# A gate part's phases summed and wrapped at its full length, a fold in two operations, a mask in one

## The chip, the cores and the metric

The kernel runs on one core of a Trainium2 chip. The metric is the device time in microseconds (us) of one execution. Its engines are TensorE (PE, matmul and transpose; its weight loads are PEld), VectorE (DVE), ScalarE (ACT), GpSimd (POOL) and SyncE (SP), which issues the DMAs. Each runs its own list of instructions in order, and they wait for one another through semaphores.

## The reference

Three stages follow one another: a gated linear attention with a complex gate, a token and channel mixer through a Fourier transform, and a second mixer with learned matrices. The change lies in the first and in the transform.

```
def _attn_ref(q, k, v, a_re, a_im):          # (4, 8, 768, 48) each
    mag = np.sqrt(a_re * a_re + a_im * a_im)
    scale = np.minimum(mag, 0.999) / (mag + 1e-06)
    a_re_n, a_im_n = (a_re * scale, a_im * scale)
    for t in range(S):
        new_re = ar * S_re - ai * S_im
        new_im = ar * S_im + ai * S_re
        S_re, S_im = (new_re + kv, new_im)
        y[:, :, t] = np.einsum('bhd,bhde->bhe', q[:, :, t], S_re)

def _moe_ref(x, w_ch1, w_ch2):               # x (4, 768, 384)
    X = np.fft.fft(np.fft.fft(x, axis=1), axis=2)
    u = x + np.real(X).astype(np.float32)
    un = (u - mean(u)) / np.sqrt(var(u) + 1e-06)
    return u + np.maximum(un @ w_ch1, 0.0) @ w_ch2

def _moe2_ref(x, w_tok1, w_tok2, w_ch1, w_ch2):
    u = x + (np.maximum(x.T @ w_tok1, 0.0) @ w_tok2).T
    return u + np.maximum(u @ w_ch1, 0.0) @ w_ch2
```

## The kernel before

The first stage works in chunks of 128 tokens. There are NM = 24 of them, six for each of four batches, numbered m, with j the place in the batch. In a chunk PE turns the keys (L1165, `turn_keys`), multiplies keys and queries into the scores of eight heads (L1173, four heads to a PSUM bank), adds to the state (L1202, `update`), and for the chunk before it multiplies the masked scores with the values (L1189) and the queries with the state (L1191). The outputs are turned (L1210, `turn_y`) and gathered into `yT`. Once a batch is whole its Fourier transform runs between the chunks: `middle` (L1219), `width_transform` (L1234) and `sequence_transform` (L1248 to L1252). `keep_busy` (L1258) issues matmuls with no use for their result: six at the very start, five in each chunk of the first batch and eight at the start of each later one. After chunk 23 come the two channel stages, whose matmuls are L233 to L235.

The gates are prepared ahead of this by ACT and DVE in nine parts, p0 to p8: p0 holds one chunk, p1 two, the others three each. A part holds 3 x 128 x chunks elements in each of 128 partitions, so 384, 768 or 1152. The magnitude of the gate gives the decays; its angle gives the phases. For the angle, ACT takes the arctangent and the sign of the real part (`arctangents`, L726 and L727) and writes with L730 into `t4` the half turn that is added where the real part is negative: 0.25 - 0.25 x sign, so 0 or 0.5. DVE (`phases`) scales the arctangent (L930) and then sums the angles over the tokens, a chunk at a time: three scans of 128 (L942), the nearest integer (L945), the difference, which is the wrapped phase (L947). The next chunk's scans start at the last value of the chunk before. L949 keeps the last value for the next part (`carry`). ACT takes the sines and cosines (`sines`, L737 to L740), and DVE multiplies keys and queries with them (`products`, L960 to L964); SP sends these out to memory and back in another layout (`turn_out`, `turn_back`), from where PE takes them.

The order on each engine is written out by hand. From p2 on, a part is spread over six chunks: squares in the first, magnitudes, inverses and factors, arctangents and phases in the fourth, sines and the first products in the fifth, the rest of the products in the sixth, with two chunks left before PE needs the part. In the fourth of these chunks `phases` stands on DVE ahead of `masked(m)`, which multiplies the scores of the chunk with the mask out of PSUM (L989, twice 512 elements), and `wait_for_outputs` makes PE wait for both halves before the next chunk's first L1189. On ACT, `arctangents` stands ahead of `keys_turned` (L746, which copies turned keys that PE needs for L1202), and `sines` ahead of it too; `magnitudes` stands ahead of `evacuate_y` (L753) and of `middle` (L765). `fold_sequence` on DVE adds and subtracts the two halves of a finished batch, for each of three groups (L1002, L1003), ahead of `width_transform`.

Of the kernel before, what the change touches and what calls it, by code (L numbers as in the profile page):

```python
# [8 lines left out]
B, H, S, D = 4, 8, 768, 48  # L9
# [3 lines left out]
P = 128  # L13
NT = S // P
KD = DM // P
# [10 lines left out]
fp32 = mybir.dt.float32  # L26
fp32r = mybir.dt.float32r
ALU = mybir.AluOpType
ACT = mybir.ActivationFunctionType
# [10 lines left out]
ROUND = 12582912.0  # L40
# [258 lines left out]
def forward(nc, ap, lay, c, u_out, x2, out, steep):  # L299
    with ExitStack() as ctx:  # L300
# [39 lines left out]
        GA = 16  # L340
        GV = [10 + 3 * p.chunks + 2 * len(PAIRS[p.n]) for p in parts]
        act0 = [GA * p.turn for p in parts]
# [67 lines left out]
        half_pi, ln_eps, ones = in_late(P, 1), in_late(P, 1), in_late(P, 1)  # L410
        least, at_floor, quarter, nearly_zero = in_late(P, 1), in_late(P, 1), in_late(P, 1), in_late(P, 1)
        bottom = in_late(P, 3 * TM)

# [23 lines left out]

        bank = [ctx.enter_context(nc.psum_tensor(f"bank{i}", [P, 512], fp32)) for i in range(8)]
        tr_bank, sc_bank, st_bank, y_bank, f_bank = bank[0:2], bank[2:4], bank[4], bank[5], bank[6:8]
# [43 lines left out]
        def products_done(p, i):  # L483
            return vec0[p.n] + 10 + 3 * p.chunks + 2 * (i // 2)

        def angles_room(p):
            return slice(2 * CT, 3 * CT) if p.n == 0 else slice(0, p.T)

# [195 lines left out]
        def _(act):  # L684
# [10 lines left out]
            def magnitudes(p):  # L695
                s, T, n = p.s, slice(0, p.T), act0[p.n]
                act.wait_ge(vec_step[s], vec0[p.n] + 1)
                A(t1_b[s][:, :, T], t1_b[s][:, :, T], ACT.Ln).then_inc(act_step[s], 1)
                act.wait_ge(act_step[s], n + 3)
                A(t2_b[s][:, :, T], t1_b[s][:, :, T], ACT.Exp, scale=-0.5, bias=ln_eps[:, 0:1]).then_inc(act_step[s], 1)  # L700
                if p.turn:
                    for m in range(parts[p.n - 2].first, parts[p.n - 2].end):
                        act.wait_ge(k_out[m % RING], 32 * (m // RING + 1))
                A(t3_b[s][:, :, T], t1_b[s][:, :, T], ACT.Exp, scale=0.5).then_inc(act_step[s], 1)
                for o in parts[max(p.n - 2, 0):p.n] if p.n > 1 else []:
                    act.wait_ge(vec_step[o.s], vec0[o.n] + 7 + 3 * o.chunks)
                A(t4[:, :, angles_room(p)], re_b[p.r][:, :, T], ACT.Abs).then_inc(act_step[s], 1)
# [15 lines left out]
            def arctangents(p):  # L723
                s, T = p.s, slice(0, p.T)
                act.wait_ge(vec_step[s], vec0[p.n] + 6)
                A(t3_b[s][:, :, T], t3_b[s][:, :, T], ACT.Arctan).then_inc(act_step[s], 1)  # L726
                A(im_b[p.r][:, :, T], re_b[p.r][:, :, T], ACT.Sign, scale=3.0,  # L727
                  bias=nearly_zero[:, 0:1]).then_inc(act_step[s], 1)
                act.wait_ge(act_step[s], act0[p.n] + 12)
                A(t4[:, :, angles_room(p)], im_b[p.r][:, :, T], ACT.Identity, scale=-0.25,  # L730
                  bias=quarter[:, 0:1]).then_inc(act_step[s], 1)

            def sines(p):
                s, T, n = p.s, slice(0, p.T), act0[p.n]
                re, im = re_b[p.r], im_b[p.r]
                act.wait_ge(vec_step[s], vec0[p.n] + 9 + 3 * p.chunks)
# [39 lines left out]

            act.wait_ge(consts_set, 4)
            logarithm_tables()
# [94 lines left out]
        def _(dve):  # L873
# [51 lines left out]
            def phases(p):  # L925
# [5 lines left out]
                                       op0=ALU.mult, op1=ALU.mult).then_inc(vec_step[s], 1)  # L931
                first = angles_room(p).start
                for i in range(p.chunks):
                    T = slice(i * CT, (i + 1) * CT)
                    offset = slice(first + i * CT, first + (i + 1) * CT)
                    dve.wait_ge(vec_step[s], n + 9 + 3 * i)
                    for g in range(3):
                        if i:
                            start = t3_b[s][:, g, i * CT - 1:i * CT]
                        else:  # L940
                            start = carry[:, 1 - s, g:g + 1] if p.j0 else 0.0
                        last = V.tensor_tensor_scan(t3_b[s][:, g, T], t3_b[s][:, g, T], t4[:, g, offset], start, ALU.add, ALU.add)  # L942
                    last.then_inc(vec_step[s], 1)
                    dve.wait_ge(vec_step[s], n + 10 + 3 * i)
                    V.tensor_scalar(re[:, :, T], t3_b[s][:, :, T], ROUND, ROUND, ALU.add, ALU.subtract).then_inc(vec_step[s], 1)  # L945
                    dve.wait_ge(vec_step[s], n + 11 + 3 * i)
                    V.tensor_tensor(t3_b[s][:, :, T], t3_b[s][:, :, T], re[:, :, T], ALU.subtract).then_inc(vec_step[s], 1)  # L947
                dve.wait_ge(vec_step[s], n + 9 + 3 * p.chunks)
                V.tensor_copy(carry[:, s, :], t3_b[s][:, :, p.T - 1]).then_inc(vec_step[s], 1)  # L949
# [68 lines left out]
            V.memset(ln_eps[:, :], LN_EPS).then_inc(consts_set, 1)  # L1018
            V.memset(quarter[:, :], 0.25).then_inc(consts_set, 1)
            V.memset(nearly_zero[:, :], 1e-20).then_inc(consts_set, 1)  # L1020
            V.memset(ones[:, :], 1.0)
# [5 lines left out]
            squared(p1)  # L1027
            dve.wait_ge(consts_set, 5)
            logs(p0)
# [1009 lines left out]
```

## Time and profile before

| | us |
|---|---|
| median of 3 runs | 1055.72 |
| lowest, highest | 1052.52, 1065.31 |
| the profiled execution's time | 1050.42 |
| its span, first to last instruction | 1048.4 |
| PE busy | 982.1 (94%) |
| PEld busy | 951.2 (91%) |
| DVE busy | 514.9 (49%) |
| ACT busy | 357.8 (34%) |
| mean granted clock of TensorE | 0.978 |

The busy shares are means over very different stretches. In the channel stages, which fill the span from about 375 us on, PE is busy all the time and DVE a quarter of it. In the attention stage before them DVE is nearly as full as PE. The granted clock is 1.00 where TensorE runs at 2.4 GHz and 0.50 where it runs at 1.2 GHz.

### The profile page before, as it was taken

The numbers are of one execution on the slowest core, as the hardware profiler recorded it, in microseconds if no ns is written. First come the engines' busy times: TensorE is split into PE (matmuls) and PEld (weight loads), VectorE is DVE, ScalarE is ACT, GpSimd is POOL, SyncE is SP. The second block draws the span as 40 slices with busy tenths as digits, with TensorE's granted clock in tenths as the row PEclk, the third lists the DMA queues.
The fourth block names the chain that finished last, engine by engine and source line by source line (L and its number), as shares of the span: only waits on it lengthen the run. The fifth ranks groups of instructions, "written<-read, shape, count | busy, mean of one in ns | idle before, by whom it ended". The sixth has DMA issues, their size and how long they took to land.

```text
span 1048.4 us, 15600 instructions
## 1 busy us (share of the span) xinstructions
PE 982.1 (94%) x6154; PEld 951.2 (91%) x6154; DVE 514.9 (49%) x940; ACT 357.8 (34%) x532; POOL 16.4 (2%) x12
## 2 busy tenths in 40 slices
PE   0389999999999999999999999999999999999997
PEld 0268889889899899999999999999999999999997
DVE  5888699999855654234324222542223214223220
ACT  7676666676531520220221221431213102121120
POOL 0000000000000000000000000030000000000000
PEclk9789899998999999999999999999999999999999
DMA  6689977986776064021021010010001001000000
GB/s 208 197 232 263 254 220 190 235 244 154 191 206 239 16 243 171 16 75 45 24 66 45 30 61 23 16 54 16 8 23 45 23 15 53 23 0 23 9 16 26
DMA packets 96745, 104.75 MB, mean 100 GB/s; under 512 B 13104, under 2 KB 90288, under 8 KB 96688
## 3 DMA queue, kind: packets, MB, share of 16 engines
q1 hardware_dynamic: 96688, 104.00, 33.6%
q8 instruction: 35, 0.57, 0.2%
q14 instruction: 22, 0.18, 0.1%
HBM read 70.86 MB, written 33.11 MB: 99 GB/s over the span
## 4 chain that ended last, share of the span: by engine, by line
PE 81%; DVE 8%; ACT 7%; issue 2%; DMA 0%; SPq 0%; DVEq 0%; ACTq 0%
PE bank L233 21%; PE bank L235 21%; PE bank L234 21%; PE bank L1173 3%; PE bank L1191 2%; DVE n_area L942 2%; PE bank L1189 2%; PE bank L1234 2%; PE bank L1250 2%; PE bank L1252 2%; PE bank L1202 2%; PE bank L1258 2%; PE bank L243 1%; DVE n_area L947 1%; DVE n_area L930 1%
## 5 line engine op out<-in xcount | busy, mean ns | idle before, releaser
L121 ACT ACTIVATE hh<-bank 128x384 fp32r<-128x384 f32 x192 | 94.5, 492 | 375.0 <-PE bank L235 375.0
L209 DVE SCALAR_TENSOR_TENSOR hl<-bank,hh 128x384 fp32r<-128x384 f32 x192 | 107.0, 557 | 195.6 <-ACT hh L121 195.6
L233 PE MATMUL bank<-w2h,hh 128*128 128x384 f32 x576 | 193.3, 336 | 0.0
L233 PE MATMUL bank<-nTh,w1h 128*128 128x384 f32 x576 | 193.0, 335 | 0.0
L235 PE MATMUL bank<-w2h,hl 128*128 128x384 f32 x576 | 192.5, 334 | 0.0
L234 PE MATMUL bank<-w2l,hh 128*128 128x384 f32 x576 | 192.5, 334 | 0.0
L235 PE MATMUL bank<-nTh,w1l 128*128 128x384 f32 x576 | 192.5, 334 | 0.0
L234 PE MATMUL bank<-nTl,w1h 128*128 128x384 f32 x576 | 192.4, 334 | 0.0
L233 PEld LDWEIGHTS bank<-nTh,w1h 128*128 128x128 f32 x576 | 108.1, 188 | 0.4 <-issue 0.2
L234 PEld LDWEIGHTS bank<-w2l,hh 128*128 128x128 f32 x576 | 108.2, 188 | 0.0
L234 PEld LDWEIGHTS bank<-nTl,w1h 128*128 128x128 f32 x576 | 108.1, 188 | 0.0
L233 PEld LDWEIGHTS bank<-w2h,hh 128*128 128x128 f32 x576 | 108.1, 188 | 0.0
L235 PEld LDWEIGHTS bank<-w2h,hl 128*128 128x128 f32 x576 | 108.1, 188 | 0.0
L235 PEld LDWEIGHTS bank<-nTh,w1l 128*128 128x128 f32 x576 | 108.1, 188 | 0.0
L1173 PE MATMUL bank<-w_area 96*128 96x128 f32 x384 | 77.8, 309 | 0.4 <-DMA w_area<-q_turn 0.4
L223 DVE TENSOR_TENSOR late_area<-bank,tok_raw 128x384 f32<-128x384 f32 x24 | 13.4, 557 | 125.1 <-PE bank L235 125.1
L1258 PE MATMUL bank<-late_area,ident 128*128 128x384 f32 x120 | 46.5, 542 | 28.2 <-DVE w_flat L961 28.2
L1189 PE MATMUL bank<-w_area 128*128 128x48 f32 x384 | 65.6, 256 | 2.3 <-DVE w_area L989 2.3
L1258 PEld LDWEIGHTS bank<-late_area,ident 128*128 128x128 f32 x120 | 24.9, 215 | 44.3 <-issue 33.2
L1191 PE MATMUL bank<-late_area,w_area 96*128 96x48 f32 x320 | 63.3, 280 | 0.0
L1189 PEld LDWEIGHTS bank<-w_area 128*128 128x128 f32 x384 | 59.0, 195 | 3.1 <-DVE w_area L989 3.1
L114 ACT ACTIVATE nTh<-bank 128x384 fp32r<-128x384 f32 x48 | 22.2, 491 | 113.4 <-PE bank L243 113.4
(156 smaller groups left out, 1294.1 us busy)
## 6 DMA issues: line engine op xcount, KB each, us to landing
w_area<-k_turn SPq DMA_DIRECT2D x24, 384.0 KB, 4.8
w_area<-q_turn SPq DMA_DIRECT2D x24, 384.0 KB, 6.1
q_turn<-w_raw SPq DMA_DIRECT2D x30, 192.0 KB, 3.0
k_turn<-n_area SPq DMA_DIRECT2D x24, 192.0 KB, 2.6
k_turn<-w_flat SPq DMA_DIRECT2D x24, 192.0 KB, 2.7
u_scratch<-h_area SPq DMA_DIRECT2D x24, 192.0 KB, 6.4
w_raw<-in_moe_w_ch SPq DMA_DIRECT2D x2, 2304.0 KB, 12.4
x_flat<-u_scratch SPq DMA_DIRECT2D x4, 1152.0 KB, 10.0
```

The costliest lines, as they stand in the source:

```text
L114: self.nc.scalar.activation(self.nTh[:, :, i * P:(i + 1) * P], self.tr_bank[i % 2][:, 0:DM].rearrange("p (k t) -> p k t", k=KD), ACT.Copy) ...
L121: self.nc.scalar.activation(self.hh[:, m, :], self.mm_bank[(g * (KF + TPG) + m) % 2][:, 0:TG], ACT.Relu).then_inc(self.h_high, 1)
L209: self.nc.vector.scalar_tensor_tensor(out=self.hl[:, m, :], in0=self.mm_bank[(g * (KF + TPG) + m) % 2][:, 0:TG], scalar=0.0, in1=self.hh[: ...
L233: self.nc.tensor.matmul(out, lh, rh, start=(n == 0), stop=False)
L234: self.nc.tensor.matmul(out, lh, rl, start=False, stop=False)
L235: last = self.nc.tensor.matmul(out, ll, rh, start=False, stop=(n == len(pairs) - 1))
L942: last = V.tensor_tensor_scan(t3_b[s][:, g, T], t3_b[s][:, g, T], t4[:, g, offset], start, ALU.add, ALU.add)
L1173: made = mm(sc_bank[h // 4][:, (h % 4) * P:(h % 4 + 1) * P], kT[:, r, h, :], qT[:, r, h, :], start=True, stop=True)
L1189: made = mm(y_bank[:, cols], pr[:, h, :], v_sb[:, p.s, m - p.first, cols], start=True, stop=not later)
L1191: made = mm(y_bank[:, cols], qT[:, m % RING, h, :], state[:, n % 3, cols], start=False, stop=True)
L1202: summed = mm(st_bank[0:HD2, cols], kt[:, h, :], v_sb[:, p.s, m - p.first, cols], start=True, stop=True)
L1258: mm(f_bank[0][:, 0:S // 2], ident[:, :], blank[:, :], start=True, stop=True)
```

## The change

Four edits are made together.

1. `phases` sums a whole part at once: three scans of up to 384, then one rounding and one difference over all elements, in place of one set of these for each chunk.
2. So that the sum does not grow over 384 tokens, the half turns have alternating sign: even tokens get 0 or +0.5, odd tokens 0 or -0.5. ACT therefore writes `t4` in two operations with a step of two elements, each half as long as the one before; the second has scale 0.25 and a bias of -0.25 (`less_quarter`, one more memset at the start).
3. `masked` reads both score banks, now one tensor of 1024 columns, in one operation, and waits for all eight heads.
4. `fold_sequence` does its three groups in one addition and one subtraction.

The counts that the waits compare with are renumbered to match.

```diff
@@ arctangents (ACT)
-                A(t4[:, :, angles_room(p)], im_b[p.r][:, :, T], ACT.Identity, scale=-0.25,
-                  bias=quarter[:, 0:1]).then_inc(act_step[s], 1)
+                room = angles_room(p)
+                A(t4[:, :, room.start:room.stop:2], im_b[p.r][:, :, 0:p.T:2], ACT.Identity, scale=-0.25, bias=quarter[:, 0:1])
+                A(t4[:, :, room.start + 1:room.stop:2], im_b[p.r][:, :, 1:p.T:2], ACT.Identity, scale=0.25,
+                  bias=less_quarter[:, 0:1]).then_inc(act_step[s], 1)
@@ phases (DVE)
-                for i in range(p.chunks):
-                    T = slice(i * CT, (i + 1) * CT)
-                    offset = slice(first + i * CT, first + (i + 1) * CT)
-                    dve.wait_ge(vec_step[s], n + 9 + 3 * i)
-                    for g in range(3):
-                        if i:
-                            start = t3_b[s][:, g, i * CT - 1:i * CT]
-                        else:
-                            start = carry[:, 1 - s, g:g + 1] if p.j0 else 0.0
-                        last = V.tensor_tensor_scan(t3_b[s][:, g, T], t3_b[s][:, g, T], t4[:, g, offset], start, ALU.add, ALU.add)
-                    last.then_inc(vec_step[s], 1)
-                    dve.wait_ge(vec_step[s], n + 10 + 3 * i)
-                    V.tensor_scalar(re[:, :, T], t3_b[s][:, :, T], ROUND, ROUND, ALU.add, ALU.subtract).then_inc(vec_step[s], 1)
-                    dve.wait_ge(vec_step[s], n + 11 + 3 * i)
-                    V.tensor_tensor(t3_b[s][:, :, T], t3_b[s][:, :, T], re[:, :, T], ALU.subtract).then_inc(vec_step[s], 1)
+                dve.wait_ge(vec_step[s], n + 9)
+                for g in range(3):
+                    start = carry[:, 1 - s, g:g + 1] if p.j0 else 0.0
+                    last = V.tensor_tensor_scan(t3_b[s][:, g, T], t3_b[s][:, g, T], t4[:, g, angles_room(p)], start, ALU.add, ALU.add)
+                last.then_inc(vec_step[s], 1)
+                dve.wait_ge(vec_step[s], n + 10)
+                V.tensor_scalar(re[:, :, T], t3_b[s][:, :, T], ROUND, ROUND, ALU.add, ALU.subtract).then_inc(vec_step[s], 1)
+                dve.wait_ge(vec_step[s], n + 11)
+                V.tensor_tensor(t3_b[s][:, :, T], t3_b[s][:, :, T], re[:, :, T], ALU.subtract).then_inc(vec_step[s], 1)
@@ masked (DVE)
-                for half in range(2):
-                    dve.wait_ge(sc_made, 2 * m + half + 1)
-                    dve.wait_ge(y_made, m)
-                    V.tensor_tensor(pr[:, 4 * half:4 * half + 4, :], sc_bank[half][:, :].rearrange("p (h t) -> p h t", h=4),
-                                    mask[:, :].rearrange("p (o t) -> p o t", o=1).broadcast_to([P, 4, P]),
-                                    ALU.mult).then_inc(sc_free, 1)
+                dve.wait_ge(sc_made, 2 * m + 2)
+                dve.wait_ge(y_made, m)
+                V.tensor_tensor(pr[:, :, :], score_banks[:, :].rearrange("p (h t) -> p h t", h=H),
+                                mask[:, :].rearrange("p (o t) -> p o t", o=1).broadcast_to([P, H, P]),
+                                ALU.mult).then_inc(sc_free, 2)
@@ fold_sequence (DVE)
-                for k_ in range(KD):
-                    fwd, back = yT[:, k_, 1:half], yT[:, k_, S - 1:half:-1]
-                    V.tensor_tensor(fold[:, 0, k_, 1:half], fwd, back, ALU.add)
-                    V.tensor_tensor(fold[:, 1, k_, 1:half], fwd, back, ALU.subtract).then_inc(folded, 1)
+                fwd, back = yT[:, :, 1:half], yT[:, :, S - 1:half:-1]
+                V.tensor_tensor(fold[:, 0, :, 1:half], fwd, back, ALU.add)
+                V.tensor_tensor(fold[:, 1, :, 1:half], fwd, back, ALU.subtract).then_inc(folded, KD)
```

The order of the instructions shows it at two places. On DVE in chunk 0, the phases of p2 and the mask behind them, before (the scans appear under the name of the instruction that carries them; n_area is `t3_b` and, for this part, `re_b`, w_area is `t4` and the masked scores, late_area holds `carry` and the mask):

```order
L930 SCALAR_TENSOR_TENSOR n_area<-n_area 128x1152
L942 SCALAR_TENSOR_TENSOR n_area<-n_area,late_area,w_area 128x128 x3
L945 TENSOR_SCALAR n_area<-n_area 128x3x128
L947 TENSOR_TENSOR n_area<-n_area 128x3x128
L942 SCALAR_TENSOR_TENSOR n_area<-n_area,w_area 128x128 x3
...
L949 COPY late_area<-n_area 128x3
L989 TENSOR_TENSOR w_area<-bank,late_area 128x512 x2
```

and of the change, at the same place:

```order
L936 SCALAR_TENSOR_TENSOR n_area<-n_area 128x1152
L941 SCALAR_TENSOR_TENSOR n_area<-n_area,late_area,w_area 128x384 x3
L944 TENSOR_SCALAR n_area<-n_area 128x1152
L946 TENSOR_TENSOR n_area<-n_area 128x1152
L948 COPY late_area<-n_area 128x3
L987 TENSOR_TENSOR w_area<-score_banks,late_area 128x1024
```

Fifteen instructions of summing and wrapping have become five, and two of masking one; nothing has changed places around them.

On ACT, the arctangents of p2 and the copies of the turned keys behind them (w_area is `t4`, then the keys), before:

```order
L726 ACTIVATE n_area<-n_area 128x1152
L727 ACTIVATE n_area<-n_area,late_area 128x1152
L730 ACTIVATE w_area<-n_area,late_area 128x1152
L746 ACTIVATE w_area<-bank 128x384 x2
```

and of the change:

```order
L730 ACTIVATE n_area<-n_area 128x1152
L731 ACTIVATE n_area<-n_area,late_area 128x1152
L735 ACTIVATE w_area<-n_area,late_area 128x576
L736 ACTIVATE w_area<-n_area,late_area 128x576
L752 ACTIVATE w_area<-bank 128x384 x2
```

One instruction of 1152 elements has become two of 576 ahead of the copies; the order is the same.

## Rows read from the trace of the kernel before

**Rows 1.** Waits of PE: who for, us in total, times, longest us.
```profile
PE bank L1202 <- ACT w_area L746: 17.3, 1, 17.3
PE bank L1165 <- ACT w_area L760: 3.9, 15, 0.3
PE bank L1189 <- DVE w_area L989: 2.3, 4, 1.1
PE bank L1234 <- DVE w_area L1003: 1.9, 1, 1.9
PE bank L1234 <- ACT late_area L765: 1.6, 2, 0.8
PE bank L1210 <- ACT h_area L753: 1.5, 2, 0.9
```
**Rows 2.** Timeline of PE: start us, us, work, idle before and its releaser.
```profile
55.55 2.76 PE L1202 MATMUL bank<-w_area 128*96 128x48 f32 x16 [17.32 <-ACT w_area L746]
64.53 0.87 PE L1189 MATMUL bank<-w_area 128*128 128x48 f32 x6 [0.81 <-DVE w_area L989]
...
99.17 0.42 PE L1189 MATMUL bank<-w_area 128*128 128x48 f32 x2 [1.05 <-DVE w_area L989]
...
204.97 0.55 PE L1210 MATMUL bank<-ident,h_area 128*128 128x128 f32 x3 [0.91 <-ACT h_area L753]
```
**Rows 3.** Timeline of PE, first L1189 and next L1210 around chunks 3 and 4.
```profile
86.50 0.35 PE L1189 MATMUL bank<-w_area 128*128 128x48 f32 x2
...
96.50 0.49 PE L1210 MATMUL bank<-ident,h_area 128*128 128x128 f32 x3
...
114.16 0.49 PE L1210 MATMUL bank<-ident,h_area 128*128 128x128 f32 x3
```
**Rows 4.** Windows: stretch, length, busy of PE, PEld, DVE, ACT, POOL, clock, DMA, GB/s.
```profile
48.00:52.00 4.00, 0.00 (x0) 0.00 (x0) 3.42 (x4) 3.94 (x4) 0.00 (x0) 0.50 1.05 324
104.00:108.00 4.00, 4.00 (x23) 4.00 (x22) 2.53 (x5) 3.97 (x5) 0.00 (x0) 0.50 1.06 385
248.00:252.00 4.00, 3.75 (x36) 3.54 (x34) 3.94 (x8) 3.35 (x4) 0.00 (x0) 1.00 0.12 44
252.00:256.00 4.00, 4.00 (x23) 4.00 (x22) 3.90 (x10) 3.94 (x6) 0.00 (x0) 0.53 0.00 0
```
**Rows 5.** Timeline of DVE, phases of p2: first scans, first rounding, carry, mask.
```profile
56.15 1.23 DVE L942 TENSOR_TENSOR_SCAN n_area<-n_area,late_area,w_area 128x128 f32<-128x128 f32 x3
57.41 0.42 DVE L945 TENSOR_SCALAR n_area<-n_area 128x384 f32<-128x384 f32 x1
...
63.11 0.17 DVE L949 COPY late_area<-n_area 128x3 f32<-128x3 f32 x1
63.19 1.29 DVE L989 TENSOR_TENSOR w_area<-bank,late_area 128x512 f32<-128x512 f32 x2
```
**Rows 6.** Instructions of DVE by line and form: count, busy us, mean ns, idle before.
```profile
L900 DVE TENSOR_TENSOR_SCAN x_flat<-x_flat,late_area 128x1152 f32<-128x1152 f32 x7 | 17.9, 2557 | 0.2
L888 DVE TENSOR_TENSOR n_area<-n_area,w_area 128x1152 f32<-128x1152 f32 x7 | 9.4, 1349 | 0.0
L945 DVE TENSOR_SCALAR w_raw<-n_area 128x384 f32<-128x384 f32 x15 | 6.4, 425 | 0.5
L900 DVE TENSOR_TENSOR_SCAN x_flat<-x_flat,late_area 128x256 f32<-128x256 f32 x3 | 1.9, 674 | 0.0
L895 DVE TENSOR_SCALAR late_area<-x_flat 128x9 f32<-128x9 f32 x7 | 1.2, 168 | 0.0
```
**Rows 7.** Instructions of ACT by line and form, the same columns.
```profile
L730 ACT ACTIVATE w_area<-w_raw,late_area 128x1152 f32<-128x1152 f32 x4 | 5.0, 1255 | 0.1
L730 ACT ACTIVATE w_area<-w_raw,late_area 128x384 f32<-128x384 f32 x1 | 0.6, 614 | 0.0
```
**Rows 8.** Timeline of DVE, the last batch's fold: first and last of six, and what follows.
```profile
350.22 0.55 DVE L1002 TENSOR_TENSOR w_area<-w_area 128x383 f32<-128x383 f32 x1
...
352.56 0.55 DVE L1003 TENSOR_TENSOR w_area<-w_area 128x383 f32<-128x383 f32 x1
```

More of the change, by code:

```diff
@@ L340, in forward @@
         GA = 16
-        GV = [10 + 3 * p.chunks + 2 * len(PAIRS[p.n]) for p in parts]
+        GV = [13 + 2 * len(PAIRS[p.n]) for p in parts]
         act0 = [GA * p.turn for p in parts]
@@ L411, in forward @@
         least, at_floor, quarter, nearly_zero = in_late(P, 1), in_late(P, 1), in_late(P, 1), in_late(P, 1)
+        less_quarter = in_late(P, 1)
         bottom = in_late(P, 3 * TM)
@@ L436, in forward @@
             xh=rounded("xh", w2_flat_at, 0, NT, DM), xl=rounded("xl", w2_flat_at, NT * DM, NT, DM))
-        bank = [ctx.enter_context(nc.psum_tensor(f"bank{i}", [P, 512], fp32)) for i in range(8)]
+        low_bank = [ctx.enter_context(nc.psum_tensor(f"bank{i}", [P, 512], fp32)) for i in range(2)]
+        score_banks = ctx.enter_context(nc.psum_tensor("score_banks", [P, 1024], fp32))
+        high_bank = [ctx.enter_context(nc.psum_tensor(f"bank{i}", [P, 512], fp32)) for i in range(4, 8)]
+        bank = low_bank + [score_banks[:, 0:512], score_banks[:, 512:1024]] + high_bank
         tr_bank, sc_bank, st_bank, y_bank, f_bank = bank[0:2], bank[2:4], bank[4], bank[5], bank[6:8]
@@ L483, in products_done @@
         def products_done(p, i):
-            return vec0[p.n] + 10 + 3 * p.chunks + 2 * (i // 2)
+            return vec0[p.n] + 13 + 2 * (i // 2)
         def angles_room(p):
@@ L705, in magnitudes @@
                 for o in parts[max(p.n - 2, 0):p.n] if p.n > 1 else []:
-                    act.wait_ge(vec_step[o.s], vec0[o.n] + 7 + 3 * o.chunks)
+                    act.wait_ge(vec_step[o.s], vec0[o.n] + 10)
                 A(t4[:, :, angles_room(p)], re_b[p.r][:, :, T], ACT.Abs).then_inc(act_step[s], 1)
@@ L735, in sines @@
                 re, im = re_b[p.r], im_b[p.r]
-                act.wait_ge(vec_step[s], vec0[p.n] + 9 + 3 * p.chunks)
+                act.wait_ge(vec_step[s], vec0[p.n] + 12)
                 A(re[:, :, T], t3_b[s][:, :, T], ACT.Abs).then_inc(act_step[s], 1)
@@ L775, in angle_tables @@
                 act.preload_act_table_set("trig_and_small")
-            act.wait_ge(consts_set, 4)
+            act.wait_ge(consts_set, 5)
             logarithm_tables()
@@ L931, in phases @@
                                        op0=ALU.mult, op1=ALU.mult).then_inc(vec_step[s], 1)
-                first = angles_room(p).start
-                for i in range(p.chunks):
-                    T = slice(i * CT, (i + 1) * CT)
-                    offset = slice(first + i * CT, first + (i + 1) * CT)
-                    dve.wait_ge(vec_step[s], n + 9 + 3 * i)
-                    for g in range(3):
-                        if i:
-                            start = t3_b[s][:, g, i * CT - 1:i * CT]
-                        else:
-                            start = carry[:, 1 - s, g:g + 1] if p.j0 else 0.0
-                        last = V.tensor_tensor_scan(t3_b[s][:, g, T], t3_b[s][:, g, T], t4[:, g, offset], start, ALU.add, ALU.add)
-                    last.then_inc(vec_step[s], 1)
-                    dve.wait_ge(vec_step[s], n + 10 + 3 * i)
-                    V.tensor_scalar(re[:, :, T], t3_b[s][:, :, T], ROUND, ROUND, ALU.add, ALU.subtract).then_inc(vec_step[s], 1)
-                    dve.wait_ge(vec_step[s], n + 11 + 3 * i)
-                    V.tensor_tensor(t3_b[s][:, :, T], t3_b[s][:, :, T], re[:, :, T], ALU.subtract).then_inc(vec_step[s], 1)
-                dve.wait_ge(vec_step[s], n + 9 + 3 * p.chunks)
+                dve.wait_ge(vec_step[s], n + 9)
[7 more added lines that the diff above has]
+                V.tensor_tensor(t3_b[s][:, :, T], t3_b[s][:, :, T], re[:, :, T], ALU.subtract).then_inc(vec_step[s], 1)
+                dve.wait_ge(vec_step[s], n + 12)
                 V.tensor_copy(carry[:, s, :], t3_b[s][:, :, p.T - 1]).then_inc(vec_step[s], 1)
@@ L1019, in _ @@
             V.memset(quarter[:, :], 0.25).then_inc(consts_set, 1)
+            V.memset(less_quarter[:, :], -0.25).then_inc(consts_set, 1)
             V.memset(nearly_zero[:, :], 1e-20).then_inc(consts_set, 1)
@@ L1027, in _ @@
             squared(p1)
-            dve.wait_ge(consts_set, 5)
+            dve.wait_ge(consts_set, 6)
             logs(p0)
```

## The prediction

> **What bounds the kernel now.** I read first who waits for whom on PE. From its second burst of work, at 55.55 us, PE stands still for little more than ten microseconds in a stage that lasts until about 350: [rows 1] hold all of it but scraps, the 17.3 us being the wait that ends at 55.55. Everything behind the attention stage is matmuls of the channel stages, which the change does not touch. So the change can bring only what stands in [rows 1], plus an earlier second burst. The timeline says where the waits are [rows 2]: 0.81 and 1.05 us before the outputs of chunks 0 and 3, for a mask that stands on DVE behind the phases of a part, and 0.91 us for ACT's copy of an output (its row in [rows 1] has 1.5 in two, so the other is 0.6). The 3.9 us in fifteen pieces are PE waiting for a transpose bank to be copied out; no edit is near them, and they stay.
>
> Then I read the clock. TensorE has 0.50, the lower of its two levels (1.2 GHz), in three stretches of some 10 to 20 us: around 40 to 61 us, while PE mostly stands still, around 102 to 112, and around 252 to 263 [rows 4]. What the second costs can be read off: from the first L1189 to the next L1210 it is 96.50 - 86.50 = 10.0 us in one chunk, and 114.16 - 99.17 = 15.0 us in the next, with the same matmuls [rows 2, 3]. A low stretch under full work costs 5.0 us, as much as all the waits that I can remove. Before the one at 102 PE had waited 1.05 us; before the one at 252 it had been 3.75 of 4.00 us busy.
>
> Last I read DVE. In the phases of p2 it takes 63.11 - 56.15 = 6.96 us from the first scan to the last wrapped chunk, and the mask of chunk 0 follows at once, at 63.19 [rows 5]. PE gets it at 64.53.
>
> **The change, part by part.** *Phases, three chunks.* A scan of 256 takes 674 ns and one of 1152 takes 2557 [rows 6], so 2.10 ns an element; one of 384 takes 674 + 128 x 2.10 = 943 ns. Three make 2.83 less the overlap; I take 2.8. The rounding at 1152 has no row. It takes 168 ns for 9 elements and 425 for 384 [rows 6], 0.685 ns an element, which gives 0.95 us; the bounds are 0.43 (length costs nothing more) and 0.425 + 768 x 1.03 = 1.22, at the pace at which L930's kind of work and L888 go (1349 ns for 1152, about 1.03 each). I take 0.95 because the line through two sizes of its own kind lies between. The difference costs 1.35 as L888 does [rows 6]. With 0.03 us between dependent steps (56.15 + 1.23 to 57.41 in [rows 5]) the sum is 5.2 us against 6.96: 1.76 less. The bounds of the rounding make it 1.5 to 2.3. There are seven such parts: 12.3 us less on DVE. *Phases, two chunks (p1).* Before: two thirds of 6.96, 4.64 us. After: three scans of 256 (2.0), 0.69 and 0.95 us, and gaps, 3.75: 0.9 less. p0 has one chunk and stays.
>
> The row of the rounding goes faster than one element in each DVE cycle. The Trainium skill says that an fp32 `tensor_scalar` out of and into SBUF runs at two elements a cycle (VectorE: DVE Perf Modes, section The perf-mode tier table). By that rule 768 more elements cost 400 ns at 0.96 GHz, an estimate of 0.83 us in place of 0.95 and 13.1 in place of 12.3 us less on DVE for the seven parts; no run here shows the long form yet.
>
> *Half turns in two.* ACT's L730 takes 1255 ns at 1152 and 614 at 384 [rows 7]: 0.835 ns an element on a fixed 0.293 us. Two of 576 take 2 x 0.774 less about 0.09 us by which neighbours overlap (the overlap on DVE, 63.11 + 0.17 against 63.19 in [rows 5]), 1.46: 0.2 more for every part, whatever its length. No row shows a step of two elements. Below, it costs nothing; above, each element could cost twice, which would add 2 x 576 x 0.835 ns = 0.96 us more to a three-chunk part. I take nothing. Behind these instructions on ACT wait the copies of turned keys (L746), for PE's L1202, and on DVE the phases.
>
> *Mask in one.* Two of 512 take 1.29 us together; one of 1024 by L888's pace some 1.22. PE needs both halves anyway. The mask now begins when all eight heads are scored, which matters only where DVE was waiting for scores: there it ends 0.5 us later than before. PE has the update, the transforms and the turns between the last score and the first masked product, and the four waits of [rows 1] for L989 are all in chunks where DVE was full, not waiting. Cost: nothing. If that cover were gone it would be 0.5 us in each of at most 24 chunks.
>
> *Fold.* Six of 383 elements take 352.56 + 0.55 - 350.22 = 2.89 us for the last batch [rows 8]; two of 1149 take 1.35 + 1.27 = 2.62. 0.27 less, four times. PE waits for it only the last time (1.9 us in [rows 1]); the others lie beside full PE work.
>
> *On the path.* (a) The second burst: the half turns of p0 put phases back 0.2, those of p1 give 0.9, the half turns of p2 take 0.2. It starts 0.5 earlier, but at the lower clock [rows 4], which ended about 61 us here; work moved into that stretch advances at half pace, so 0.25 us. (b) The masks: 2.3 us in four waits, the largest 1.05. Phases end 1.76 - 0.2 = 1.56 us earlier than now relative to PE, so all go: 2.3. (c) L765: 1.6 us in two waits of 0.8. There ACT is late because its sines waited for phases; 1.56 covers 0.8: 1.6. (d) L753: 1.5 in two waits, for the same reason (at 204.97 through a DVE that had been full since the part before): 1.5. (e) The last fold: 0.27. Sum: 0.25 + 2.3 + 1.6 + 1.5 + 0.27 = 5.9 us. Next late, after these, is ACT's copy of a transpose bank, the 3.9 us that stay. Of some 14 us that DVE gives up, most turns into DVE idling.
>
> The profiled execution took 1050.42 us; 5.9 less is 1044.5. The median of the three runs is 5.3 above it, about one low-clock stretch more. Runs scatter by such steps, so I set the middle of the four executions, (1052.52 + 1055.72) / 2 = 1054.1, as the base: 1048.
>
> **The rivals.** *A low stretch goes too (22%).* The one at 102 us followed PE's 1.05 us wait, which (b) removes. If the wait was its cause, 5.0 us more are saved: 1043. Against it: the stretch at 252 came without such a wait. The Trainium skill describes matmuls that drop to the lower clock after idle gaps between bursts (TensorE: Matmul & The Clock Gate, section HAM oscillation); by that rule fewer waits would mean fewer drops, and the trace agrees in one place of two.
>
> *The gain is not passed on (17%).* PE, early by a wait, meets the next late thing: keys and queries coming back through memory while DMA is full (1.05 in [rows 4]), or ACT, which has 0.2 us more in each part. Then only (a), (e) and some of (b) stay, about 2 us: 1052. For it: in chunks with arctangents ACT is nearly full. Against it: [rows 1] hold no wait for a DMA in this stretch at all, and the products leave earlier, not later.
>
> *More low stretches: slower (15%).* Where a low stretch falls seems to hang on how work lies in time, and the change moves all of it. Each costs 5.0 us; from the second extra one on, they outweigh the 5.9: 1054.1 - 5.9 + 10 = 1058. For it: the highest run is 12.8 us over the lowest, two to three such steps. Against it: PE idles less than before.
>
> *Strided writes at half pace (4%).* Then the half turns cost 1.2 in place of 0.2 us in each part. (a) becomes a loss of about 1 us, and phases end only 0.6 earlier, so that half of (b) to (d) stays: 1052.
>
> **How the numbers follow.** The forecast as summed: 42%, 1048, own range 1044 to 1052 for the scatter of the base. With 22% at 1043, 21% at 1052 and 15% at 1058, a range of 1039 to 1058 leaves out about 2 in 10: a low stretch less and a fast base below, the slow rival's upper half above. It takes in the rounding's and the stride's bounds, which move the sum by less than 2 us. A change of 2%, about what a measurement of this kernel can tell from none, is 21 us: below 1034.6 or above 1076.8. The removable waits sum to 6 us, so only three or four low stretches fewer, or more, could do it: faster 3%, slower 2%, within 2% 95%.
>
> **What would show it.** In the changed kernel's profile: phases from first scan to the carry's copy at 5.2 us for three chunks; the two halves of the half turns at 0.77 us each; no PE wait for the mask, and none for L753's and L765's counterparts over 0.3 us; the last fold 0.27 us shorter. PE's second burst at about 55.1. Low-clock stretches: three, or two with none near 100 us. I am wrong if the mask waits stay, if the half turns take over 1 us each, if a wait for returned keys appears, or if the time is over 1055 with the waits gone and the clock no lower than before.

## The result

The changed kernel takes 1045.16 us in the median of 20 runs (1036.84 to 1059.2), the kernel before 1058.09 us in the median of 20 (1048.13 to 1070.35). The ratio is 0.9873, 95% interval 0.9847 to 0.9899. The medians differ by 12.9 us, where 6 were forecast. The ratio would make it 13.4, because it leaves out the slow runs, those over 1.5% above a kernel's fastest, among them five of the changed kernel's; the table and the means below take all. The time lies in the forecast's range, 2.8 us below the 1048 that was named. That is luck in part, for two errors stand against each other: the base, set at 1054.1, was 4 us too low, and the gain was twice the sum.

The profiled execution of the changed kernel is one of its slowest (1057.98 us, span 1056.0, mean clock 0.966). The waits of its profile are of use, its length is not. What makes it long can be read off all runs, since each lists its mean granted clock: the changed kernel's 20 run from 1059.2 us at 0.966 to 1037.0 us at 0.987, 1.03 us for each 0.001 of clock. Of the time that TensorE spends at 1.2 GHz instead of 2.4, half is lost if PE has work; over a run that is (1 - mean clock) x span, the "low-clock loss". Taking it off gives a time at full clock. It scatters by 1 to 2.4 us from run to run (standard deviation; 3.6 in e9). It is an accounting, not a measurement: the stretch that each execution has while PE idles near 45 us, and the one at its end, are taken off as if they cost all they could, alike for all kernels; a low stretch that lies under a wait of PE is overrated. The kernel before, measured on four chips beside the experiments, had 1027.0 to 1027.9 us. So I trust differences of more than about 1 us.

| kernel | runs | median us | low-clock loss, mean us | time less loss, us |
|---|---|---|---|---|
| before, all runs beside the experiments | 87 | 1058.8 | 31.0 ± 0.6 | 1027.3 ± 0.2 |
| the change | 20 | 1045.2 | 24.7 ± 1.7 | 1022.5 ± 0.3 |

The means differ by 1058.2 - 1047.2 = 11.0 us: 4.8 at full clock, and 6.3 ± 1.8 in time at the lower clock. (The ± are standard errors.)

Waits of PE in the changed kernel's profile, who for, us in total, times, longest us, to be read against [rows 1]:

```profile
PE bank L1200 <- ACT w_area L752: 16.6, 1, 16.6
...
PE bank L1163 <- DMA w_area<-k_turn: 1.8, 1, 1.8
...
PE bank L1208 <- ACT h_area L759: 0.9, 1, 0.9
PE bank L1232 <- DVE w_area L1000: 0.6, 1, 0.6
```

The waits for the mask (2.3 us) and for ACT's middle row (1.6 us) are gone. One of two waits for ACT's copy of an output stays. A wait that was not there has come: 1.8 us for the keys of chunk 6, coming back through memory.

DVE's timeline of the phases of p2 and the mask behind, to be read against [rows 5], and one row of p1 ahead of it:

```profile
33.16 0.69 DVE L944 TENSOR_SCALAR w_raw<-n_area 128x768 f32<-128x768 f32 x1
...
56.61 2.83 DVE L941 TENSOR_TENSOR_SCAN n_area<-n_area,late_area,w_area 128x384 f32<-128x384 f32 x3
59.48 0.76 DVE L944 TENSOR_SCALAR n_area<-n_area 128x1152 f32<-128x1152 f32 x1
60.27 1.36 DVE L946 TENSOR_TENSOR n_area<-n_area 128x1152 f32<-128x1152 f32 x1
61.67 0.17 DVE L948 COPY late_area<-n_area 128x3 f32<-128x3 f32 x1
61.78 1.22 DVE L987 TENSOR_TENSOR w_area<-score_banks,late_area 128x1024 f32<-128x1024 f32 x1
```

From the first scan to the carry's copy it is 61.67 - 56.61 = 5.06 us; it was 6.96.

And where the clock falls. PE's timeline around chunk 6, and the windows there (columns as in [rows 4]):

```profile
118.35 0.88 PE L1163 MATMUL bank<-ident,w_area 96*128 96x96 f32 x8 [1.79 <-DMA w_area<-k_turn]
```
```profile
120.00:124.00 4.00, 4.00 (x24) 4.00 (x23) 3.09 (x3) 3.69 (x6) 0.00 (x0) 0.59 0.94 260
128.00:132.00 4.00, 4.00 (x22) 3.69 (x21) 3.19 (x6) 0.74 (x2) 0.00 (x0) 0.50 0.82 62
```

The stretch of [rows 4] near 102 us is not there; one of 13.7 us begins at 120.7, 2.4 us after PE's new wait ended.

### The profile page after: what moved, and what is told of

Same layout as the page of the kernel before. It is cut to its first block, busy times and chain, and to the rows that moved or that the text cites. A ratio compares the mean times of both kernels' runs of the same rounds, so it can differ in the third digit from the quotient of the medians.

```text
span 1056.0 us, 15471 instructions
## 1 busy us (share of the span) xinstructions
PE 993.3 (94%) x6154; PEld 961.8 (91%) x6154; DVE 500.1 (47%) x826; ACT 360.8 (34%) x541; POOL 16.4 (2%) x12
## 4 chain that ended last, share of the span: by engine, by line
PE 87%; ACT 5%; DVE 4%; DMA 2%; issue 2%; SPq 0%; DVEq 0%; ACTq 0%
PE bank L233 21%; PE bank L235 20%; PE bank L234 20%; PE score_banks L1171 4%; PE bank L1256 3%; PE bank L1200 3%; PE bank L1189 3%; PE bank L1187 3%; PE bank L1232 3%; PE bank L1248 2%; PE bank L1250 2%; PE score_banks L243 1%; PE bank L1163 1%; PE bank L1246 1%; DMA k_turn<-w_flat 1%
## 5 line engine op out<-in xcount | busy, mean ns | idle before, releaser
L1171 PE MATMUL score_banks<-w_area 96*128 96x128 f32 x384 | 79.9, 316 | 0.3 <-DMA w_area<-q_turn 0.3
L1256 PE MATMUL bank<-late_area,ident 128*128 128x384 f32 x120 | 49.0, 566 | 29.3 <-DVE w_flat L960 29.3
L223 DVE TENSOR_TENSOR late_area<-bank,tok_raw 128x384 f32<-128x384 f32 x24 | 13.4, 557 | 125.1 <-PE bank L235 125.1
L1189 PE MATMUL bank<-late_area,w_area 96*128 96x48 f32 x320 | 64.8, 286 | 0.0
L114 ACT ACTIVATE nTh<-score_banks 128x384 fp32r<-128x384 f32 x48 | 22.2, 491 | 113.3 <-PE score_banks L243 113.3
```

Of the source, the lines that this page charges most:

```text
L114: self.nc.scalar.activation(self.nTh[:, :, i * P:(i + 1) * P], self.tr_bank[i % 2][:, 0:DM].rearrange("p (k t) -> p k t", k=KD), ACT.Copy) ...
L1171: made = mm(sc_bank[h // 4][:, (h % 4) * P:(h % 4 + 1) * P], kT[:, r, h, :], qT[:, r, h, :], start=True, stop=True)
L1189: made = mm(y_bank[:, cols], qT[:, m % RING, h, :], state[:, n % 3, cols], start=False, stop=True)
L1256: mm(f_bank[0][:, 0:S // 2], ident[:, :], blank[:, :], start=True, stop=True)
```

## The experiments

Theory A: the waits that were summed make the smaller part of the gain, and the rest is less time at the lower clock. Rival B: the waits were under-counted. A second question came with the first answer. Theory P: low stretches follow pauses of PE. Rival Q: they fall at random. Every kernel ran beside the kernel before on one chip.

| kernel | runs | median us | loss, mean us | time less loss, us | ratio, 95% interval |
|---|---|---|---|---|---|
| e1 before again | 12 | 1058.1 | 30.7 ± 1.7 | 1027.4 ± 0.3 | 0.9995 (0.9958 to 1.0033) |
| e2 phases only | 6 | 1044.6 | 20.5 ± 1.6 | 1023.9 ± 0.4 | 0.9886 (0.9843 to 0.9930) |
| e3 mask and fold only | 12 | 1055.5 | 32.3 ± 1.7 | 1025.8 ± 0.4 | 1.0005 (0.9973 to 1.0037) |
| e4 DVE time put back | 12 | 1055.7 | 28.1 ± 2.0 | 1027.4 ± 0.7 | 0.9987 (0.9954 to 1.0021) |
| e5 half turn in one | 6 | 1046.7 | 21.6 ± 2.9 | 1022.1 ± 0.4 | 0.9888 (0.9816 to 0.9961) |
| e6 less busy | 6 | 1047.4 | 30.5 ± 2.2 | 1016.5 ± 0.4 | 0.9899 (0.9847 to 0.9951) |
| e7 busy moved | 12 | 1047.4 | 23.0 ± 1.6 | 1023.6 ± 0.4 | 0.9926 (0.9886 to 0.9965) |
| e8 keys back first | 12 | 1050.5 | 27.7 ± 1.4 | 1022.6 ± 0.3 | 0.9953 (0.9911 to 0.9994) |
| e9 before, mask first | 6 | 1070.0 | 34.5 ± 3.3 | 1034.2 ± 1.5 | 1.0142 (1.0078 to 1.0207) |
| e10 busy before chunk 6 | 7 | 1046.7 | 21.6 ± 0.7 | 1024.8 ± 0.5 | 0.9904 (0.9868 to 0.9939) |
| e11 both busy edits | 12 | 1048.6 | 20.0 ± 1.8 | 1026.8 ± 0.4 | 0.9883 (0.9845 to 0.9922) |
| e12 gates later | 12 | 1043.3 | 22.2 ± 2.0 | 1022.9 ± 0.7 | 0.9875 (0.9837 to 0.9913) |

### Two parts of the gain

**e1**, the kernel before, unchanged.

> The kernel before, unchanged, to get the granted clock of each of its runs beside its time. The runs of the changed kernel list a mean clock from 0.966 to 0.987, and their times fall with it from 1059.2 to 1036.8 us. Theory A (the summed waits are the smaller part of the gain; the rest is fewer stretches of TensorE at 1.2 GHz): at an equal mean clock this kernel is 4 to 7 us slower than the changed one, and its mean clock over the runs is lower than the changed kernel's by 0.004 to 0.008. Rival B (the waits were under-counted): at an equal clock it is 11 to 14 us slower, with the same mean clock.

At full clock it is 4.9 us slower than the change, and it loses 6.1 ± 2.4 us more to the low clock. Both numbers are A's; B's 11 to 14 at equal clock is out.

### Which edit it was

**e2**, only the phases and half turns; `masked`, the banks and `fold_sequence` as before.

> Of the change only the phases at full length, with the alternating half turns; mask and fold as before. Theory A: nearly all of the gain, ratio to before 0.985 to 0.992, since the waits for mask and ACT come from the phases; the last fold's 0.27 us is missing. Rival (mask and fold matter, since each instruction less on a full DVE counts): ratio 0.993 or more.

**e3**, only the mask and the fold:

```diff
-                for half in range(2):
-                    dve.wait_ge(sc_made, 2 * m + half + 1)
+                dve.wait_ge(sc_made, 2 * m + 2)
...
+                ALU.mult).then_inc(sc_free, 2)
```

> Of the change only the mask in one operation and the fold in two; phases and half turns as before. Theory A: 0.3 to 1.5 us less, ratio 0.997 to 1.001. Rival (mask and fold matter): ratio 0.995 or less. Rival (the mask, begun only after all eight heads, makes PE wait): ratio over 1.002 and a longer wait for the mask than 2.3 us.

The phases alone have the ratio of the whole change. The mask and fold alone cannot be told from nothing; at full clock they give 1.5 us and the phases 3.4, which add up to the 4.8 of both within their errors. The loss to the low clock goes with the phases too: every kernel with fast phases and all its keeping-busy matmuls has lost less in the mean (20.0 to 27.7 us) than the kernels without (28.1 to 34.5). The mask that starts only after eight heads made no wait: PE's waits for it are 1.4 us in e3's profile against 2.3 in [rows 1].

**e4**, the changed kernel with DVE's time put back, by scans whose result the rounding overwrites:

```diff
+                for g in range(p.chunks - 1):
+                    V.tensor_tensor_scan(re[:, g, T], t3_b[s][:, g, T], t4[:, g, angles_room(p)], 0.0, ALU.add, ALU.add)
                 for g in range(3):
```

> The changed kernel with DVE's time given back: ahead of the long scans of each three-chunk part, two more scans of 384 whose result is overwritten by the rounding (one of 256 for the two-chunk part), some 1.8 us for each part. Nothing else differs. Theory A (what counts is how early DVE is done with the phases): the gain is gone, ratio 0.997 to 1.004, and the waits for the mask and for ACT's copies are back within 0.5 us of their totals before. Rival (a gain from fewer instructions, or from the place of the work in time, that does not hang on DVE's time): ratio 0.993 or less.

The gain is gone, also at full clock (1027.4 ± 0.7 against 1027.3). Waits of PE in its profile:

```profile
PE bank L1189 <- DVE w_area L989: 3.4, 5, 1.1
PE bank L1234 <- ACT late_area L771: 1.7, 2, 0.8
PE bank L1234 <- DVE w_area L1002: 1.6, 1, 1.6
PE bank L1210 <- ACT h_area L759: 1.5, 2, 0.9
```

They are back: 1.7 and 1.5 us as in [rows 1], and the mask's even 1.1 us over it. So the gain of the phases comes through how early DVE is done with them, and not through the number of instructions. Whether the mask and the fold bring their 1.5 us without it stays open: e4 has both, and is 1.6 ± 0.8 us slower at full clock than e3. The wait for the mask of chunk 3 is back at 1.09 us, and 2.6 us behind it a low stretch of 10.2 us begins, as in [rows 2, 4].

**e5**, the half turn in one ACT instruction, of one sign:

```diff
-                A(t4[:, :, room.start:room.stop:2], im_b[p.r][:, :, 0:p.T:2], ACT.Identity, scale=-0.25, bias=quarter[:, 0:1])
-                A(t4[:, :, room.start + 1:room.stop:2], im_b[p.r][:, :, 1:p.T:2], ACT.Identity, scale=0.25,
-                  bias=less_quarter[:, 0:1]).then_inc(act_step[s], 1)
+                A(t4[:, :, angles_room(p)], im_b[p.r][:, :, T], ACT.Identity, scale=-0.25,
+                  bias=quarter[:, 0:1]).then_inc(act_step[s], 1)
```

> The changed kernel with the half turns written by one ACT instruction again, all of one sign, so that the sum runs up to 192 over a part and is rounded more coarsely; all else as changed. Tells the price of the split. Theory A: the pair costs 0.2 us more than the one on ACT in each part, and as the waits behind it are gone, only the start of PE's second burst shows it: the time without what the low clock costs falls from 1022.5 by 0 to 0.6 us. Rival (ACT is nearly full where the arctangents stand, and each of nine parts passes its 0.2 on): it falls by 1.5 us or more.

0.4 ± 0.5 us less at full clock: the split costs next to nothing, as forecast.

### Whether pauses bring the low clock

**e9**, the kernel before, with the mask ahead of the phases:

```diff
                 if (m, 3) in stage_at:
+                    masked(m)
                     phases(stage_at[m, 3])
```

> The kernel before with one edit: in chunks with phases the mask stands ahead of them on DVE. The waits for the mask go although not a microsecond of DVE's work does. Tells whether the low stretch near 102 us, which stood in three profiled kernels that have PE's 1.05 us wait for the mask at 99 us, comes from that wait. Theory P: no low stretch begins between 99 and 108 us, 2.3 us of waits are gone, and the loss to the low clock falls from 31 to 24 to 28 us in the mean; ratio 0.990 to 0.996. Rival Q (random): loss stays at 31, ratio 0.997 to 1.000, since phases now end 1.2 us later.

The waits for the mask fall from 2.3 to 0.6 us, but the phases now end later, and the time is 1.4% longer. P's forecast of a loss of 24 to 28 us failed (34.5 ± 3.3), and so did both ratios. This was more of an intervention than I had meant, so it says little on P. Waits of PE in its profile:

```profile
PE bank L1204 <- ACT w_area L746: 19.3, 2, 17.2
PE bank L1204 <- issue: 4.4, 5, 1.8
...
PE bank L1250 <- DVE h_area L1015: 2.1, 2, 1.0
```

PE waits some 6 us more before L1204, the state's update, and 2.1 before the transform, all for what stands behind the later phases. Of the two orders, the kernel's own is the better. No low stretch begins between 99 and 108 us, but 3 begin from 76 to 149 us, each after a pause of 1.1 us or more.

**e7**, two of five keeping-busy matmuls moved behind the turned keys:

```diff
+                if 0 < m <= NCH:
+                    keep_busy(2)
                 if m:
                     wait_for_outputs(m - 1)
...
-                    keep_busy(5)
+                    keep_busy(3)
```

> The changed kernel; of the five matmuls that keep TensorE busy in each chunk of the first batch, two stand behind the turning of the next chunk's keys, not with the others. The same work. Tells whether the low stretches of the first batch come from the pause around the turns. Theory P (low clock follows a pause of PE by a few us): no low stretch between 65 and 150 us but one after a wait for returned keys, and the runs lose under 22 us to the low clock in the mean. Rival Q (they fall at random): as the changed kernel, 24.7 us lost.

A loss of 23.0 ± 1.6 against 24.7 ± 1.7 does not decide it, and is not under P's 22. The profile has the longest of the pauses at chunk 6:

```profile
118.16 0.88 PE L1163 MATMUL bank<-ident,w_area 96*128 96x96 f32 x8 [2.58 <-DMA w_area<-k_turn]
118.87 1.48 PE L1256 MATMUL bank<-late_area,ident 128*128 128x384 f32 x4
```

No low stretch begins behind it, and this is the only one of the fourteen profiles with none from 65 us to the end of the attention stage. So a pause need not bring one. The two moved matmuls stand right behind this pause; whether they are why nothing follows is not shown.

**e8**, fetching back ahead of the next sending out:

```diff
                     turn_out(first)
-                    turn_out(first + 1)
                     turn_back(first)
+                    turn_out(first + 1)
                     turn_back(first + 1)
```

> The changed kernel with one edit on SP: the first chunk of a part is fetched back before the second is sent out. In the changed kernel PE waits 1.8 us for chunk 6's keys at 118 us, and a low stretch of 13.7 us begins 2 us later. Theory P (a pause of PE brings the low stretch): the wait is gone, the stretch near 120 us too, and the time falls by 4 to 8 us against the changed kernel's 1045.2, to 1037 to 1041, with a mean loss to the low clock of 16 to 20 us. Rival Q (stretches at random): only the 1.8 us go, 1043. Rival (SP, held up until the queries have landed, sends the second chunk too late): a longer wait at the second chunk, 1045 or more.

All three theories missed. The wait stays, at 1.9 us, and so does the stretch, from 118.7 us. The keys' sending out had landed only when SP could have fetched them in either order, so the order on SP was not what made them late.

**e10**, five more keeping-busy matmuls ahead of the wait:

```diff
-                    keep_busy(5)
+                    keep_busy(10 if m == NCH - 1 else 5)
```

> The changed kernel with ten instead of five keeping-busy matmuls in chunk 5, 1.65 us more work, ahead of the turning of chunk 6's keys. In four of the five profiled kernels with fast phases PE waits 1.8 to 2.3 us for these keys and a low stretch of 13.7 or 17.1 us begins 1 to 2 us later. Theory P (the pause brings the low stretch): the wait is under 0.7 us, no low stretch begins between 112 and 130 us, the mean loss to the low clock is 17 to 21 us in place of 24.7, and the time without it stays within 0.7 us of 1022.5; so 1038 to 1042 in all. Rival Q (at random): the same loss, 24.7, and a time of 1045 to 1048.

Windows around chunk 6 in e10, and then in e8 for comparison:

```profile
116.00:120.00 4.00, 3.88 (x17) 2.31 (x16) 2.82 (x3) 0.42 (x2) 0.00 (x0) 1.00 1.06 301
120.00:124.00 4.00, 3.87 (x35) 3.87 (x36) 0.14 (x1) 3.97 (x6) 0.00 (x0) 1.00 0.89 253
```
```profile
116.00:120.00 4.00, 2.99 (x24) 2.99 (x24) 2.21 (x3) 3.97 (x6) 0.00 (x0) 0.83 1.02 275
120.00:124.00 4.00, 4.00 (x21) 4.00 (x21) 3.93 (x5) 2.21 (x3) 0.00 (x0) 0.50 0.65 153
```

With the pause filled with work, the clock stays at 1.00, in e10 as P says. The loss is 21.6 ± 0.7, 3.0 less than the change's with an error of 1.8, which leans P's way and proves nothing alone. The time, 1046.7 us, is what Q named: at full clock the kernel is 2.3 us slower, which uses it up. The price of the five matmuls had been forecast at half its size. PE's timeline in chunk 5, the change and then e10:

```profile
112.84 3.39 PE L1256 MATMUL bank<-late_area,ident 128*128 128x384 f32 x10
```
```profile
112.60 6.62 PE L1256 MATMUL bank<-late_area,ident 128*128 128x384 f32 x20
```

Each keeping-busy matmul stands in the trace as two pieces, so five take 3.3 us and not 1.65; less the wait of 1.8 us that leaves 1.5 of the 2.3.

**e11**, both edits of e7 and e10.

> The changed kernel with two keeping-busy matmuls of each first-batch chunk moved behind the next chunk's turned keys, and five more in chunk 5. Theory P: no low stretch from 65 to 130 us, loss 16 to 20 us, 1037 to 1042 in all, the best so far if the two edits add. Rival Q: loss near 23 to 25 us, time 1046 or more.

The lowest loss of all, 20.0 ± 1.8 (e2 has 20.5 ± 1.6), and no low stretch from 65 to 151 us, as P says. But it is paid for with 4.3 us at full clock, so the forecast of the best time failed: 1048.6.

**e6**, three keeping-busy matmuls instead of five.

> The changed kernel with three instead of five keeping-busy matmuls in each chunk of the first batch, 0.7 us less work in each of six. Theory P: PE reaches every hand-over earlier, so waits for DVE, ACT and returned keys grow in the first batch to 4 us or more, and low stretches come with them: a loss of 27 us or more, a time of 1046 to 1054. Rival Q: 3 us less work and no more low stretches, 1042 to 1044.

At full clock it is 6.0 us faster than the change, and it loses 5.8 ± 2.8 us more to the low clock. That is P's forecast of the loss. Q's time of 1042 to 1044 is not quite out: the ratio's interval reaches down to some 1044. Waits of PE in its profile:

```profile
PE bank L1208 <- ACT h_area L759: 2.8, 2, 1.9
...
PE bank L1187 <- DVE w_area L987: 1.2, 2, 0.7
```

The 1.9 us wait is new, and 2.5 us behind it a low stretch of 13.7 us begins. At 0.65 us for each matmul, 7.8 us of work were taken out, and not 4 as had been forecast. In the means over all runs nothing of it is left: 1047.0 us against 1047.2, with an error of some 3.

**e12**, the gates of parts 5 to 8 fetched later:

```diff
-                    if p.n > 3 and p.first == m + 9:
+                    if p.n > 3 and p.first == m + (9 if p.n == 4 else 7):
```

> The changed kernel with the gates of parts 5 to 8 fetched two chunks later: for part 5 behind the sending out and fetching back of part 3's first two chunks, not ahead of it. The same bytes. In the changed kernel the first keys of chunk 6 are handed to DMA at 105 us and have landed by 113, with 2.3 MB of loads issued ahead of them from 96 us. Theory D (DMA load makes these keys late, and the wait for them is the changed kernel's new bound at this place): the wait of 1.8 us is gone or under 0.5 us, and with it the low stretch at 120 us: 1037 to 1042. Rival (the late gates hold up ACT's squares, and behind them its copies of outputs): new waits for L759 over 1 us each, 1047 to 1055. Rival (the sending out itself is slow): the wait stays at 1.5 us or more, 1045.

Waits of PE in its profile:

```profile
PE bank L1208 <- issue: 2.2, 1, 2.2
...
PE bank L1163 <- DMA w_area<-k_turn: 0.2, 1, 0.2
```

Theory D holds for the wait: with the loads out of the way the keys are there, 0.2 us in place of 1.8. Its time, 1037 to 1042, did not come. The first rival holds too: the gates reach ACT late, its squares wait for them, and behind these its copy of an output makes PE wait 2.2 us one chunk later; as that wait ends, at 125.0 us, a low stretch of 3.4 us begins. The one wait replaced the other. 1043.3 us has the change's ratio (0.9875 against 0.9873); it does not beat it.

### All fourteen profiles together

Between 65 and 390 us the profiles have 45 low stretches. In the 5 us before 25 of them PE had pauses of together 0.5 us or more; of all other times in these profiles 7% have as much before them (1 to 17% in one profile). Fourteen more had only smaller pauses, most of them the 0.25 to 0.3 us between the two halves of the turned keys, 3 us before the stretch. Six had none.

Two places repeat from kernel to kernel. Four profiles have the wait of 1.0 to 1.1 us for the mask of chunk 3 (before, e1, e3, e4), and in each a low stretch begins 1.3 to 3.2 us behind it; in the ten others none begins from 90 to 112 us. Five have a pause of 1.8 to 2.6 us for the keys of chunk 6, and behind four of them a stretch begins. But of all 49 single pauses of 0.75 us or more outside low stretches, only 23 had a stretch beginning within them or in the 5 us behind.

And the place is not left to chance: the change, e6 and e11 have stretches that begin at 154.8, 209.4, 233.3 and 352.8 us, at 148.8, 203.4, 227.3 and 346.8, and at 151.4, 206.0, 229.9 and 349.4, so at the same distances. Q as put, "at random", is out. P is well supported as a tendency and is not a full account: half of the longer pauses bring nothing, the small ones are in every chunk, and some stretches have none before them. What decides stays open.

## Why the prediction came out as it did

**By its own signs.** Of what was named as showing it wrong, one came: a wait for returned keys. Two more signs failed: ACT's copy of an output is waited for 0.9 us, where at most 0.3 was named, and PE's second burst begins at 56.01 us and not at 55.1, since the first began 1.1 us later than in the profile before (29.3 against 28.2). And the profile has six low stretches and one at the end, where two or three were named.

**Scans, difference, mask, fold: right.** Three scans take 2.83 us (2.8), the difference 1.36 (1.35), the mask 1.22 (1.22), two of a fold 1.35 each.

**Rounding: the term was too large.** 0.76 us, where I took 0.95 by a line through 9 and 384 elements. The 384 are three pieces of 128, and the 1152 are one piece. As three pieces of 256 the same instruction takes 0.69 us, so the longer one costs 0.07 more. The rule of the Trainium skill that I set beside it (VectorE: DVE Perf Modes, section The perf-mode tier table) gave an estimate of 0.83. For the one long piece the trace agrees with its two elements a cycle: by it 1152 elements are 600 ns at 0.96 GHz, which leaves 160 of the 760 ns, about the 168 ns of the nine-element row.

**Half turns: slightly small.** The pair takes 0.73 to the second's start and 0.8 for that: some 1.52 us against 1.46. Strides of two elements cost little, 0.82 us for 576 elements where 0.77 was taken, so that rival is out:

```profile
L735 ACT ACTIVATE w_area<-w_raw,late_area 128x576 f32<-128x576 f32 x4 | 3.3, 824 | 0.1
```

**(a) the second burst:** the wait before it is 16.6 us against 17.3 (16.4 to 16.9 in all profiles with the new phases, 17.2 to 17.5 without), so it comes 0.7 us closer to the first. Right in kind. **(b) masks, (c) L765:** both zero, right, and e4 shows that they hang on DVE's time. **(e) the fold:** 1.9 has become 1.6 in e7, e10 and e12, right; the 0.6 above lies under a low stretch, from 352.8 us. **(d) L753: half wrong.** Of 1.5 us 0.9 stays, in chunk 12. I put it down to a DVE that had been full; but by the timelines PE there already waits for ACT before the state's update, and ACT's squares then stand between the copied keys and the copy of the output. PE and ACT move together, and the distance between them cannot shrink:

```profile
206.84 1.53 PE L1200 MATMUL bank<-w_area 128*96 128x48 f32 x16 [0.17 <-issue]
209.27 0.77 PE L1208 MATMUL bank<-ident,h_area 128*128 128x128 f32 x3 [0.91 <-ACT h_area L759]
```

**A wait I had argued away came.** "[rows 1] hold no wait for a DMA in this stretch at all" was true of the kernel before, and I read it as slack. Two things used the slack up. The kernel before came to the keys of chunk 6 at 123.4 us, 5.0 of them owed to its low stretch from 102 to 112 us; the change comes at 116.6. And the keys, which in the kernel before were fetched at 111.5 us and landed 4.9 later, at 116.4, landed at 118.3 in the change, 1.8 us later, because their sending out landed that much later. So the low stretch alone did not hide a wait: 5.0 us sooner, at 118.4, the kernel before would still have found its keys. Why the sending out was later, with the same loads ahead of it, no run shows; e12 shows that it hangs on these loads. The sum at full clock came to 4.8 us, for 5.9 forecast.

**The clock: the step that failed in size.** I let low stretches scatter about a fixed mean and gave a rival 22% to lose one. In the mean over the runs the change lost 6.3 ± 1.8 us less to them, 1.3 stretches of 5.0 us, more than all its waits. What I had for it, one pause before one stretch and none before the other, was too little to forecast by, but it pointed this way. The Trainium skill's rule (TensorE: Matmul & The Clock Gate, section HAM oscillation) that idle gaps between bursts bring the lower clock, there gaps longer than the pauses here, fits what e4, e10 and the fourteen profiles show; against it stand the six stretches that no wait went before, and the 26 longer pauses that none followed. The rival on the other side, more low stretches and a slower kernel, did not come in the mean, though the profiled execution is one with more.

**The base.** Four executions of a kernel that scatters by 22 us from fastest to slowest gave 1054.1; 87 give 1058.8. A mean clock beside each time would have shown which they were.

## What to carry to other kernels

Where one engine's clock tends to fall after pauses, a wait can cost more than its length: here about 5 us less at full clock went with 6.3 ± 1.8 us less of low-clock loss. That the second followed from the first is likely and not shown. Compare such kernels by the time left when (1 - mean clock) x span is taken off, which a dozen runs give to some 0.5 us, and by the loss itself, which they give only to 2. And a wait that a profile does not show is not slack by itself: read when the data landed and when the engine came for it, and take off what a slow stretch added.

## What the runs showed of the hardware

- A `tensor_scalar` of fp32 in SBUF takes 0.42 us for 3 pieces of 128, 0.69 for 3 of 256, but 0.76 for 1152 in one piece. So 384 elements more cost 0.27 us in the first step and 0.07 in the second, where the form changed too.
- Filling a pause of 1.8 us of PE with unneeded matmuls (e10) kept the clock at 2.4 GHz where it fell to 1.2 in four of the five other profiles that have this pause. Taking such work away (e6) gave 6.0 us at full clock and lost 5.8 ± 2.8 to the low clock.
- A hand-over through memory lands later behind loads issued ahead of it. In the change 2.3 MB of loads were issued from 8 us before the keys' sending out; its second half, issued at 105.2 us, landed at 113.2. With 1.2 MB of them moved behind (e12), it was issued at 102.8 and landed at 109.1, 6.3 us after in place of 8.0, and PE's wait fell from 1.8 to 0.2 us.
